# Low parts of wk on VectorE, the second k turned straight after outB, and v loads issued from GpSimd

## The chip, the cores and the metric

One core of one Trainium2 chip runs the whole program. The metric is the device time of one execution in microseconds.

## The reference, cut to what matters

All of it is float32. Eight batches of 576 tokens go through three blocks in a row.

```python
def sm_attn(qq, kk, vv):                       # per batch and head, head_dim 64, 8 heads
    s = scale * qq @ kk.T
    a = exp(s - max(s)); a = a / (sum(a) + 1e-9)
    return a @ vv
p_packed = sm_attn(p, k, v)                    # p: 32 packed queries per head
x = sm_attn(q, p_packed, p_packed)             # [8, 576, 512]
x_prev = shift x by one token
xk = mu_k * x + (1 - mu_k) * x_prev            # the same with mu_r for xr
kk = relu(xk @ w_k)                            # 512 -> 1024
x = sigmoid(xr @ w_r) * (kk * kk @ w_v)        # 1024 -> 512
u = x + (x^T U V)^T                            # U, V of rank 32 over the 576 tokens
out = u + relu(u @ w_ch1) @ w_ch2              # 512 -> 2048 -> 512
```

## The kernel before, in words

Every large matmul is made from three passes over split operands: a value is kept as a high part (rounded to the faster format, written by ScalarE) and a low part (the value minus the high part, one subtraction on VectorE or GpSimd), and hi*hi, hi*lo and lo*hi are accumulated (L883, L908, L922).

The engines run fixed lists of items, in the same order on each engine; an item does on an engine what it has to do there, and semaphores join them (`everything`, L1423).

**First items** (`first_items`, L190). Attention of batch 0 alone: k turned on TensorE (`k0`), then the steps `scores1`, `a`, `pv`, `pp`, `scores2`, `sm1`, `norm0`, `norm1`, `outA`, `outB`. `scores2` and `sm1` turn the second scores of two halves of the heads, take maxima and subtract them on VectorE (L795 to L801), ScalarE takes the exponential (L737); `norm0` and `norm1` sum, invert, scale and turn (L806 to L817) for the matmuls of `outA` and `outB` (L713), whose results are copied into x by ScalarE and VectorE (L743, L823). Between these steps the high parts of the weights of the second block are cast by ScalarE (items `w`, L1804), one chunk of 128x1024 at a time, from five staging slots: 10 chunks, 4 of wk, 2 of wr, 4 of wv. GpSimd makes the low part of each in four pieces (L1707), then loads the next chunk into the free slot (`load_w`, L1682). After `outB` come the mix of x and its shifted copy (L848, L861), its split (L873, L880), and `k1`: the rows of k of batch 1, loaded by SyncE, are turned on TensorE (L556, L563) and copied by ScalarE and VectorE (L618, L632). TensorE also runs filler transposes of the identity whose result nobody reads (`idle_turns`, L1742), as many as the table IDLE_TURNS (L80) says: 24 at the start, 112 after `scores2` and 36 after `outB` of batch 0.

**Second block with attention beside it.** Four pairs of batches, three chunks of 384 tokens each. A chunk is 17 slots (L61): 8 groups `k`, 3 groups `r`, 6 halves `v`, each of 12 matmuls. The attention steps of coming batches are laid into slots by tables (`batch_plans`, L98): in the first pair, those of batch 1 by the table `second`, of batches 2 and 3 by `third` and `fourth`. The first `k` group waits until all low parts of wk exist, the first `r` group for two chunks more, the first `v` group for all ten (L1763). After each group, ScalarE and VectorE empty the bank and square, split or multiply (L943, L932, L972, L960, L956, L983). A finished x2 tile is turned by VectorE (L991) and stored to a scratch in DRAM by SyncE, four issues a tile (L1605); x2 tiles 0 and 2 of a chunk go through one buffer, so the turn of tile 2 waits for the store of tile 0 (L990).

Loads stand in the same item lists, on SyncE's queue: k and q of a coming batch (L1467), p (L1474), and `load_v` (L1476) one batch ahead: ten issues, eight heads and four tails gathered in two, placed one slot after the `pv` step (L683) that reads the old rows, for which it waits.

GpSimd's list (L1697 to L1736): the low parts of the ten chunks, `scale_p` (L1676) for each batch, and in between the early pieces of the third block's weights: load a piece (L1385 to L1391), which waits for VectorE's low part of the piece before, and make its sums (L1397 to L1402); ScalarE then casts it at a fixed slot (`e_hi`, L1414), VectorE makes the low part (L1419), SyncE stores it.

**Third block.** Five column pairs of tokens; per pair two halves g, each with a stage of products into the hidden layer (L1178) and a stage of products out of it (L1266), by a scheme with seven products (R11 to T4) in three banks a side. Between products VectorE adds what a bank holds to acc (`dve_sum`, L1323). At the end of a pair eight tiles are turned by VectorE (`dve_turn_out`, L1343) and stored by SyncE, at the very end by SyncE and ScalarE. In the last stage of all, acc of two tiles is first added into the bank of product T4 (`dve_last`, L1305), TensorE's T4 waits for that (L1263), and the last two turns read the bank itself.

Of the kernel before, what the change touches and what calls it, by code (L numbers as in the profile page):

```python
# [78 lines left out]

IDLE_TURNS = {"first": 24, (0, "scores2"): 112, (0, "outB"): 36}  # L80

# [16 lines left out]
def batch_plans(kind):  # L98


    if kind == FIRST:
        third = batch_slots(15, 17, 20, 22, 23, 24, 25, 26, 28, 29, 31, 34, 36)
        fourth = batch_slots(37, 38, 40, 42, 43, 44, 45, 46, 47, 49, 50, 53, 55)
    else:
        third = batch_slots(6, 8, 11, 13, 15, 16, 17, 19, 21, 23, 25, 28, 30)
        fourth = batch_slots(32, 33, 35, 37, 38, 39, 40, 42, 45, 47, 50, 53, 55)
    here = (3, {at: steps for at, steps in fourth.items() if at < CHUNKS * NSLOT})
    rest = (1, {at - CHUNKS * NSLOT: steps for at, steps in fourth.items() if at >= CHUNKS * NSLOT})
    if kind == FIRST:
        second = {0: ("scores1",), 2: ("a",), 4: ("pv", "qA"), 5: ("qB",), 7: ("pp",), 8: ("scores2",),  # L110
                  9: ("sm1", "norm0"), 10: ("norm1",), 12: ("outA",), 13: ("outB",)}
        return [(1, second), (2, third), here]
    return [rest, (2, third), here] if kind == MIDDLE else [rest]
# [76 lines left out]
def first_items():  # L190

    items = [("start_loads",), ("p0",), ("k0",)]
    nw = 0
    for step in UNIT_STEPS[UNIT_STEPS.index("scores1"):]:
        if step in ("qA", "qB"):
            continue
        items.append(("attn", 0, step))
        if step == "scores1":
            items += [("load_k1",), ("load_p", 1), ("load_z", 1, 2), ("load_z", 1, 3)]
        elif step == "pv":  # L200
            items += [("load_v", 1), ("q0", 1)]
        elif step == "pp":
            items.append(("q0_tails",))
        elif step == "norm1":
            items.append(("omu",))
        elif step == "a":
            items.append(("q0", 0))
        for _ in range(WEIGHTS_AFTER.get(step, 0)):
            items.append(("w", nw))
            nw += 1  # L210
    items += [("mix", 0, 0), ("split", 0, 0), ("k1",)] + [("w", i) for i in range(nw, NWA - 2)]
    items += [("attn", 1, "p"), ("load_p", 2)]
    return items
# [49 lines left out]

def last_stage(p, g):

    return p == NB - 1 and g == NG - 1


def pair_plan(p, left, turns):
# [3 lines left out]
    for g in range(NG):  # L273
# [27 lines left out]
        for e in range(NPROD * NU):  # L301
# [10 lines left out]
            if i == NU - 1 and pos == R11:  # L312
                items += [("seed", g, 0), ("seed", g, 1)]
            elif i == NU - 1:
                if not (pos == T4 and last_stage(p, g)):
                    ready += [[("sum", p, g, SUM_AT[one])] for one in READY[pos]]
                if g == NG - 1 and pos in (R21, T3, R22):
                    pair = TILES[2 * (pos - R21):2 * (pos - R21) + 2]
                    done = [[("turn", p, TILES.index(t)), ("out", p, TILES.index(t))] for t in pair]
                    if p == NB - 1:  # L320
                        ready += done
                    else:
                        turns += done
            if last_stage(p, g) and pos == R22 and i in (1, 2):
                items.append(("last", i - 1))
            if g == NG - 1 and p < NB - 1 and e in US_AT:
# [29 lines left out]
class Attention:  # L356


    def __init__(self, sb, sem, scope):
# [26 lines left out]
        self.k1_act, self.k1_dve = sem("k1_act"), sem("k1_dve")  # L386
        self.v0_in, self.v1_in, self.v_in = sem("v0_in"), sem("v1_in"), sem("v_in")
        self.kq_ok, self.p_scaled, self.pT_ok = sem("kq_ok"), sem("p_scaled"), sem("pT_ok")
# [13 lines left out]
def build(nc, q, k, v, p, mu_k, mu_r, w_k, w_v, w_r, u, vv, w1, w2, out):  # L402
# [89 lines left out]
    w_in = [sem(f"w_in{i}") for i in range(RA)]  # L492
    w_hi, w_lo = sem("w_hi"), sem("w_lo")
    scaled_prev, mix_ok, x_hi, x_lo = sem("scaled_prev"), sem("mix_ok"), sem("x_hi"), sem("x_lo")
# [24 lines left out]
    hid_hi, hid_lo = sem("b_hid_hi"), sem("b_hid_lo")  # L519
    sum_ok, turn_ok, last_ok = sem("b_sum_ok"), sem("b_turn_ok"), sem("b_last_ok")  # L520
    out_done = [sem(f"b_out_done{i}") for i in range(2)]
# [122 lines left out]
    def pe_attn(pe, n, step):  # L644
# [29 lines left out]
        elif step == "pv":  # L674
            if n < 2:
                pe.wait_ge((L.v0_in, L.v1_in)[n], 16 * 3)
            else:
                pe.wait_ge(L.v_in, VLOADS * 16 * (n - 1))
            for hp in range(2):
# [185 lines left out]
    def act_split(act, C, which, sides=(0, 1)):  # L865
        if not (isinstance(C, int) and C == 0):
            act.wait_ge(moe_ps, MOE_GROUPS * (C - 1) + (KR if which else NFA))
        if isinstance(C, int) and C == 0 and which == 1:
            act.wait_ge(w_lo, NWA - 2)
        for side_ in sides:  # L870
# [63 lines left out]
    def act_group(act, C, c, slot):  # L934
# [11 lines left out]
        else:  # L946
# [5 lines left out]
            if isinstance(C, int) and C == 0 and at == 0:  # L952
                act.wait_ge(u_split, 1)
                act.wait_ge(w_lo, NWA)
            ge(act, x2s_lo, TPC * (C - 1) + at + 1)
# [289 lines left out]
    def pe_m2(pe, p, g, pos, i):  # L1245
# [6 lines left out]
        if i == 0:  # L1252
# [6 lines left out]
            else:  # L1259
                read = {T3: T2, R22: T1, T4: T3}[pos]  # L1260
                pe.wait_ge(sum_ok, base + SUM_AT[READY[read][-1]] + 1)
                if pos == T4 and last_stage(p, g):
                    pe.wait_ge(last_ok, 2)  # L1263
        for j in range(2):
# [32 lines left out]

    def dve_last(dve, j):

        p, st, w = NB - 1, 2 * (NG * NB - 1) + 1, PAIRS_B[NB - 1][1]  # L1300
        dve.wait_ge(sum_ok, sum_no(p, NG - 1, SUM_AT["22", "X", j]) + 1)
        dve.wait_ge(sum_ok, sum_no(p, 0, SUM_AT["21", "X", j]) + 1)
        nt, half = sum_place("21", j)
        to = role(st, j, "X")[:, 0:w]
        nc.vector.tensor_tensor(to, to, acc[p % 2][:, nt, half, 0:w], ALU.add).then_inc(last_ok, 1)  # L1305

    def sum_place(out_, j):
# [17 lines left out]
    def dve_turn_out(dve, p, k):  # L1325
        w = PAIRS_B[p][1]
        out_, j = TILES[k]
        no = len(TILES) * p + k
        if k >= 6 and p == NB - 1:
            dve.wait_ge(prod_ps, entry(p, NG - 1, T4, NU - 1, 1) + 1)  # L1330
        else:
            dve.wait_ge(sum_ok, sum_no(p, NG - 1, SUM_AT[(out_, LAST_SUM[out_], j)]) + 1)
        if no == 0:
# [5 lines left out]
        nt, half = sum_place(out_, j)  # L1339
        src = acc[p % 2][:, nt, half, 0:w]  # L1340
        if k >= 6 and p == NB - 1:
            src = role(2 * (NG * p + NG - 1) + 1, j, "X")[:, 0:w]
        nc.vector.transpose(blocks(turn_place(p, k)), blocks(src)).then_inc(turn_ok, 1)  # L1343

# [130 lines left out]

    def load_v(eng, n):  # L1476
        ge(eng, att.pv_ps, n)
        for h in range(VLOADS):
            if h < H:
                src = v[n, h, 0:1, :]  # L1480
                rows = bass.AP(src.tensor, src.offset, [[(TT - 1) * D, 4], [KB * D, 32], [1, (TT - 1) * D]])
                eng.dma_start(att.vn[:, h, 0:TT - 1, :].rearrange("p t d -> p (t d)"), rows).then_inc(att.v_in, 16)  # L1482
            else:
                quad = h - H
                src = v[n, :, :, :].rearrange("h (i m) d -> i h m d", m=KB)[:, :, 4 * (TT - 1) + quad, :]
                eng.dma_start(att.vn[32 * quad:32 * quad + 32, :, TT - 1, :], src).then_inc(att.v_in, 16)

# [21 lines left out]
    def load_attn(eng, kind, n, part):  # L1509
# [5 lines left out]
        elif kind == "load_v":  # L1515
            if n == 1:
                eng.wait_ge(att.pv_ps, 1)
                load_first_v(eng, n)
            else:
                load_v(eng, n)  # L1520
        else:
# [140 lines left out]
    def _(pool):  # L1662
# [26 lines left out]
        for i, m in enumerate((mu_k, mu_r)):  # L1689
# [6 lines left out]
                       u[TAIL:S, :].rearrange("(t p) r -> p t r", p=P)).then_inc(const_in, 16)  # L1696
        for i in range(NWA):  # L1697
            _, dst, a = w_chunks[i]
            pool.wait_ge(w_hi, i + 1)
            if i == CT:  # L1700
                scale_p(1)
            if i == CT:
# [7 lines left out]
            if i + RA < NWA:  # L1710
                pool.wait_ge(w_lo, i + 1)
                load_w(i + RA)
# [6 lines left out]
        for k in range(len(FIRST_AT)):  # L1719
            early_piece(k)  # L1720
            if k == 0:
                scale_p(3)
        scale_p(4)
        for g in range(1, PAIRS - 1):
            for k in range(len(EARLY_AT)):
                early_piece(early_no(g, k))
                if k == 2:
                    scale_p(2 * g + 3)
            if 2 * g + 4 < B:
                scale_p(2 * g + 4)  # L1730
        for n in range(EARLY, PIECES):
# [9 lines left out]
    def _(pe):  # L1741
# [9 lines left out]
        def first(item):  # L1751
            if item[0] in ("p0", "k0", "q0", "q0_tails", "k1"):
                pe_first(pe, *item)
            elif item[0] == "attn":
                pe_attn(pe, item[1], item[2])
                idle_turns(IDLE_TURNS.get(item[1:], 0))

        def do_a(item, g, c):
            C = CHUNKS * g + c
            if item[0] in ("k", "r", "v"):  # L1760
                if isinstance(C, int) and C == 0 and item[1] == 0:

                    pe.wait_ge(w_lo, {"k": CT, "r": CT + CT // 2, "v": NWA}[item[0]])  # L1763
                pe_group(pe, C, c, item)
# [97 lines left out]
    def _(dve):  # L1862
# [4 lines left out]
        def first(item):  # L1867
# [6 lines left out]
            elif item[0] == "split":  # L1874
                dve_split(dve, 0, item[1])
            elif item[0] == "omu":
                dve.wait_ge(const_in, 96)
# [37 lines left out]
        def do_b(item, p):  # L1915
# [4 lines left out]
            elif item[0] == "sum":  # L1920
                dve_sum(dve, *item[1:])
            elif item[0] == "last":
                dve_last(dve, item[1])
            elif item[0] == "turn":
# [33 lines left out]
```

## Time and profile before

| | us |
|---|---|
| three runs: median (lowest to highest) | 1359.19 (1357.71 to 1361.4) |
| the profiled execution | 1359.9 |
| its span in the trace | 1358.1 |
| TensorE busy | 1318.2 (97%) |
| VectorE busy | 955.9 (70%) |
| ScalarE busy | 703.8 (52%) |
| GpSimd busy | 209.0 (15%) |
| mean granted TensorE clock, share of full speed | 0.993 |

The second block runs from about 49 us to 606, the third to the end. A row of a timeline gives start and duration of an operation or of a merged run of equal ones, and in brackets how long its engine sat idle before it and what released it. SPq and POOLq are the issues of SyncE's and GpSimd's queues. A row that begins with a stretch (215.90:222.10) gives its length and then, within it, the busy time and instructions of PE, PEld (TensorE's weight loads), DVE (VectorE), ACT (ScalarE) and POOL (GpSimd), the granted TensorE clock as a share of 2.4 GHz, the busy share of the DMA engines and GB/s.

### The profile page before, as it was taken

How to read it: one execution, taken by the hardware profiler on the slowest of the kernel's cores; microseconds unless marked ns; L12 is line 12 of the kernel's file. 1: busy time of each engine (PE TensorE's matmuls, PEld its weight loads, DVE VectorE, ACT ScalarE, POOL GpSimd, SP SyncE). 2: the span in 40 equal slices, each digit the busy share in tenths (PEclk: the TensorE clock that was granted, in tenths of full speed). 3: DMA queues.
4: the chain of work that ended last, by engine and by line, in shares of the span. 5: the costliest groups of instructions: out<-in, count | busy, mean ns of one | idle time of the engine just before them, and what ended most of it. 6: DMA issues, size and time to landing. Idle time of an engine off the chain costs nothing.

```text
span 1358.1 us, 21513 instructions
## 1 busy us (share of the span) xinstructions
PE 1318.2 (97%) x7686; PEld 1134.8 (84%) x7686; DVE 955.9 (70%) x1553; ACT 703.8 (52%) x1235; POOL 209.0 (15%) x294
## 2 busy tenths in 40 slices
PE   8889998999999999999999999999999999999997
PEld 7868877888888888888999999888888888888886
DVE  5787977787877877674568676847587566856556
ACT  4656554555555556543545554645355544645352
POOL 6621021322022203412002002000030003000000
PEclk9999998999999999999999999999999999999999
DMA  9645574757465613965888899787867887678766
GB/s 242 141 87 88 132 156 95 155 146 158 98 140 137 161 24 92 282 181 148 264 261 258 261 269 318 238 241 205 240 184 201 249 225 213 190 207 214 218 190 127
DMA packets 433496, 252.50 MB, mean 186 GB/s; under 512 B 309776, under 2 KB 353840, under 8 KB 433392
## 3 DMA queue, kind: packets, MB, share of 16 engines
q1 hardware_dynamic: 422768, 238.20, 65.6%
q0 software_dynamic: 4016, 11.82, 2.7%
q10 hardware_dynamic: 6608, 1.11, 0.5%
q8 instruction: 62, 1.02, 0.3%
q14 instruction: 42, 0.34, 0.1%
HBM read 201.25 MB, written 49.81 MB: 185 GB/s over the span
## 4 chain that ended last, share of the span: by engine, by line
PE 72%; DVE 13%; SPq 7%; issue 3%; DMA 3%; ACT 2%; POOL 1%; DVEq 0%; ACTq 0%; POOLq 0%
PE bank L1178 25%; PE bank L1266 25%; PE bank L923 7%; PE bank L909 6%; PE bank L888 4%; SPq L1467 3%; SPq L1482 2%; DVE mixed L861 2%; DVE square L972 1%; DVE k_lo L960 1%; SPq L1605 1%; DVE kqT L767 1%; DVE xr_lo L880 1%; PE bank L1745 1%; PE bank L1005 1%
## 5 line engine op out<-in xcount | busy, mean ns | idle before, releaser
L1266 PE MATMUL bank<-hid_parts,w_ring 128*128 128x512 f32 (+1 forms) x1680 | 355.0, 370 | 5.7 <-issue 2.3
L1178 PE MATMUL bank<-u_parts,w_ring 128*128 128x512 f32 (+1 forms) x1680 | 353.9, 368 | 0.8 <-DVE hid_raw L1223 0.8
L1266 PEld LDWEIGHTS bank<-hid_parts,w_ring 128*128 128x128 f32 x1680 | 304.9, 188 | 54.3 <-issue 13.1
L1178 PEld LDWEIGHTS bank<-u_parts,w_ring 128*128 128x128 f32 x1680 | 304.9, 188 | 40.6 <-issue 1.3
L1289 ACT ACTIVATE hid_parts<-hid_raw 128x512 fp32r<-128x512 f32 (+1 forms) x280 | 164.8, 589 | 143.2 <-PE bank L1266 142.3
L1295 DVE TENSOR_TENSOR hid_parts<-hid_raw,hid_parts 128x512 fp32r<-128x512 f32 (+1 forms) x280 | 179.9, 646 | 72.2 <-ACT hid_parts L1289 68.5
L909 PE MATMUL bank<-xk_hi,wk_hi 128*128 128x384 f32 x384 | 132.5, 345 | 0.9 <-DVE x L983 0.8
L909 PE MATMUL bank<-xk_lo,wk_hi 128*128 128x384 f32 x384 | 129.5, 337 | 0.0
L909 PE MATMUL bank<-xk_hi,wk_lo 128*128 128x384 f32 x384 | 129.4, 337 | 0.0
L923 PE MATMUL bank<-wv_hi,k_hi 128*128 128x512 f32 x288 | 113.7, 395 | 0.2 <-ACT x L956 0.2
L923 PE MATMUL bank<-wv_lo,k_hi 128*128 128x512 f32 x288 | 112.2, 390 | 0.0
L923 PE MATMUL bank<-wv_hi,k_lo 128*128 128x512 f32 x288 | 112.1, 389 | 0.0
L943 ACT ACTIVATE square<-bank 128x384 f32<-128x384 f32 x96 | 47.0, 490 | 115.9 <-PE bank L909 89.2
L972 DVE TENSOR_TENSOR square<-square 128x384 f32<-128x384 f32 x96 | 55.6, 579 | 59.7 <-ACT square L943 59.5
L1102 POOL TENSOR_TENSOR u_sums<-acc 128x512 f32<-128x512 f32 (+1 forms) x10 | 12.1, 1214 | 503.0 <-DVE acc L1090 503.0
L1223 DVE TENSOR_TENSOR hid_raw<-bank,hid_z 128x512 f32<-128x512 f32 (+1 forms) x40 | 25.5, 638 | 85.1 <-PE bank L1178 82.8
L909 PEld LDWEIGHTS bank<-xk_hi,wk_hi 128*128 128x128 f32 x384 | 72.8, 190 | 12.1 <-issue 4.7
L1323 DVE TENSOR_TENSOR acc<-bank,acc 128x512 f32<-128x512 f32 (+1 forms) x118 | 73.1, 630 | 7.1 <-PE bank L1266 7.0
L861 DVE SCALAR_TENSOR_TENSOR mixed<-x,mu,mixed 128x384 f32<-128x384 f32 x96 | 57.2, 657 | 28.0 <-ACT mixed L848 27.9
L909 PEld LDWEIGHTS bank<-xk_lo,wk_hi 128*128 128x128 f32 x384 | 72.7, 189 | 1.1
L909 PEld LDWEIGHTS bank<-xk_hi,wk_lo 128*128 128x128 f32 x384 | 72.6, 189 | 0.0
L923 PEld LDWEIGHTS bank<-wv_hi,k_hi 128*128 128x128 f32 x288 | 54.0, 188 | 16.1 <-issue 4.0
(176 smaller groups left out, 1929.7 us busy)
## 6 DMA issues: line engine op xcount, KB each, us to landing
w_ring<-w_parts SPq DMA_DIRECT2D x560, 256.0 KB, 3.7
w_parts<-early_out SPq DMA_DIRECT2D x23, 896.0 KB, 5.1
x_scratch<-x SPq DMA_DIRECT2D x144, 64.0 KB, 2.1
kq_parts<-in_q SPq DMA_DIRECT2D x112, 72.0 KB, 2.4
w_parts<-piece_out SPq DMA_DIRECT2D x9, 896.0 KB, 4.6
kq_parts<-in_k SPq DMA_DIRECT2D x96, 72.0 KB, 2.8
v_rows<-in_v SPq DMA_DIRECT2D x49, 128.0 KB, 5.5
x_tiles<-x_scratch SPq DMA_DIRECT2D x6, 1024.0 KB, 7.1
```

The source lines that it names most:

```text
L861: last = nc.vector.scalar_tensor_tensor(out3, segments(c, ft, 0), mu[:, which, ft:ft + 1], out3, ALU.mult, ALU.add)
L888: last = nc.tensor.matmul(bank, a, b_, start=(done == 0), stop=(done == 3 * n_terms - 1))
L909: last = nc.tensor.matmul(bank[:, 0:CHUNK], wk[a][:, ct, at * P:(at + 1) * P], xk[b_][:, ct, :], start=(ct == 0 and a == 0 and b_ == 0), s ...
L923: last = nc.tensor.matmul(bank, k2[a][:, f, at * P:(at + 1) * P], wv[b_][:, f, :], start=(f == 0 and a == 0 and b_ == 0), stop=(f == NFA - ...
L943: nc.scalar.activation(square[:, at % 2, :], bank[:, 0:CHUNK], ACT.Relu).then_inc(k_ev, 1)
L972: nc.vector.tensor_tensor(square[:, at % 2, :], square[:, at % 2, :], square[:, at % 2, :], ALU.mult).then_inc(squared, 1)
L1178: last = nc.tensor.matmul(to, wring[:, e % RW, ct, a, :], uc[:, pos, b, ct, 0:w], start=(pos in FRESH and ct == 0 and a == 0 and b == 0), ...
L1266: last = nc.tensor.matmul(role(st, j, BANK_OF[pos])[:, 0:w], wring[:, e % RW, j, a, :], hid[:, no % RH, b, 0:w], start=(pos in FRESH and i ...
L1289: nc.scalar.activation(hid[:, no % RH, 0, 0:w], raw[:, pos, i, 0:w], ACT.Copy).then_inc(hid_hi, 1)
L1295: nc.vector.tensor_tensor(hid[:, no % RH, 1, 0:w], raw[:, pos, i, 0:w], hid[:, no % RH, 0, 0:w].bitcast(F32), ALU.subtract).then_inc(hid_l ...
L1323: nc.vector.tensor_tensor(to, role(st, j, name)[:, 0:w], to, ALU.add).then_inc(sum_ok, 1)
L1467: eng.dma_start(part[32 * quad:32 * quad + 32, :, :], src).then_inc(done, 16)
```

## The change

It has these parts. The low parts of wk move from GpSimd to VectorE: four subtractions of 128x1024 as items `wk_lo`, after `pp`, `norm1`, `outA` and `outB` of batch 0, with a semaphore of their own; GpSimd only waits for each and loads the next chunk. The fillers after `outB` go, so that `k1` follows `outB` on TensorE at once; 24 fillers stand behind `k1`, and the 112 after `scores2` become 104. In the table of batch 1 the steps from `scores2` on come one slot later. The v rows of batches 3 to 7 are issued from GpSimd's queue: batch 3 after the first early piece, batch 4 after the fourth, batches 5 and 7 after the fourth piece of their pair, batch 6 after the eighth, before `scale_p`. The addition of acc into the bank in the last stage goes: its sums are made as in every other stage, and the last two turns read acc.

```diff
-IDLE_TURNS = {"first": 24, (0, "scores2"): 112, (0, "outB"): 36}
+IDLE_TURNS = {"first": 24, (0, "scores2"): 104, "k1": 24}
...
-        second = {0: ("scores1",), 2: ("a",), 4: ("pv", "qA"), 5: ("qB",), 7: ("pp",), 8: ("scores2",),
-                  9: ("sm1", "norm0"), 10: ("norm1",), 12: ("outA",), 13: ("outB",)}
+        second = {0: ("scores1",), 2: ("a",), 4: ("pv", "qA"), 5: ("qB",), 7: ("pp",), 9: ("scores2",),
+                  10: ("sm1", "norm0"), 11: ("norm1",), 13: ("outA",), 14: ("outB",)}
...
         elif step == "pp":
-            items.append(("q0_tails",))
+            items += [("q0_tails",), ("wk_lo", 0)]
         elif step == "norm1":
-            items.append(("omu",))
+            items += [("wk_lo", 1), ("omu",)]
+        elif step in ("outA", "outB"):
+            items.append(("wk_lo", 2 + int(step == "outB")))
...
             elif i == NU - 1:
-                if not (pos == T4 and last_stage(p, g)):
-                    ready += [[("sum", p, g, SUM_AT[one])] for one in READY[pos]]
+                ready += [[("sum", p, g, SUM_AT[one])] for one in READY[pos]]
...
-            if last_stage(p, g) and pos == R22 and i in (1, 2):
-                items.append(("last", i - 1))
...
-                if pos == T4 and last_stage(p, g):
-                    pe.wait_ge(last_ok, 2)
...
-        if k >= 6 and p == NB - 1:
-            dve.wait_ge(prod_ps, entry(p, NG - 1, T4, NU - 1, 1) + 1)
-        else:
-            dve.wait_ge(sum_ok, sum_no(p, NG - 1, SUM_AT[(out_, LAST_SUM[out_], j)]) + 1)
+        dve.wait_ge(sum_ok, sum_no(p, NG - 1, SUM_AT[(out_, LAST_SUM[out_], j)]) + 1)
...
-    def load_v(eng, n):
+    def load_v(eng, n, done):
...
-            else:
-                load_v(eng, n)
+            elif n == 2:
+                load_v(eng, n, att.v2_in)
...
-        for i in range(NWA):
+        for i in range(CT):
+            pool.wait_ge(wk_lo_ok, i + 1)
+            load_w(i + RA)
+        scale_p(1)
+        for i in range(CT, NWA):
             _, dst, a = w_chunks[i]
             pool.wait_ge(w_hi, i + 1)
-            if i == CT:
-                scale_p(1)
             if i == CT:
                 pool.wait_ge(x_lo, 2)
...
             early_piece(k)
             if k == 0:
                 scale_p(3)
+                load_v(pool, 3, att.v_in)
+        load_v(pool, 4, att.v_in)
         scale_p(4)
         for g in range(1, PAIRS - 1):
             for k in range(len(EARLY_AT)):
                 early_piece(early_no(g, k))
                 if k == 2:
                     scale_p(2 * g + 3)
+                if k == 3:
+                    load_v(pool, 2 * g + 3, att.v_in)
             if 2 * g + 4 < B:
+                load_v(pool, 2 * g + 4, att.v_in)
                 scale_p(2 * g + 4)
...
             if item[0] in ("p0", "k0", "q0", "q0_tails", "k1"):
                 pe_first(pe, *item)
+                idle_turns(IDLE_TURNS.get(item[0], 0))
...
-                    pe.wait_ge(w_lo, {"k": CT, "r": CT + CT // 2, "v": NWA}[item[0]])
+                    if item[0] == "k":
+                        pe.wait_ge(wk_lo_ok, CT)
+                    else:
+                        pe.wait_ge(w_lo, {"r": CT // 2, "v": NWA - CT}[item[0]])
...
+            elif item[0] == "wk_lo":
+                i = item[1]
+                dve.wait_ge(w_hi, i + 1)
+                nc.vector.tensor_tensor(wk[1][:, i, :], stage_a[i], wk[0][:, i, :].bitcast(F32),
+                                        ALU.subtract).then_inc(wk_lo_ok, 1)
```

## Rows read from the trace of the kernel before

**Rows 1.** The page's busy times, share of the span and instructions of each engine.
```profile
PE 1318.2 (97%) x7686; PEld 1134.8 (84%) x7686; DVE 955.9 (70%) x1553; ACT 703.8 (52%) x1235; POOL 209.0 (15%) x294
```

**Rows 2.** The timeline of all engines, 23 to 49 us.
```profile
23.37 12.45 PE L1745 MATMUL bank<-ident 128*128 128x128 f32 x112
...
27.72 2.33 DVE L801 TENSOR_TENSOR probs<-probs,tok_max 128x576 f32<-128x576 f32 x1
...
30.75 2.55 DVE L809 TENSOR_SCALAR tok_sum<-tok_sum 128x18 f32<-128x18 f32 x1
...
38.56 0.75 PE L713 MATMUL bank<-kqT,packed 32*64 32x288 f32 x16 [2.74 <-DVE kqT L817]
...
40.99 5.82 PE L1745 MATMUL bank<-ident 128*128 128x128 f32 x36
...
45.42 1.95 DVE L880 TENSOR_TENSOR xk_lo<-mixed,xk_hi 128x768 fp32r<-128x768 f32 x2
...
48.87 0.45 PE L909 MATMUL bank<-xk_hi,wk_hi 128*128 128x384 f32 x1
```

**Rows 3.** Two lines' instructions on VectorE: shortest, median and longest duration in ns.
```profile
L801 DVE TENSOR_TENSOR probs<-probs,tok_max x16: 757/758/2332, 25.1 to 491.3; 128x576 f32<-128x576 f32 x16
...
L809 DVE TENSOR_SCALAR tok_sum<-tok_sum x16: 175/177/2547, 30.8 to 504.5; 128x18 f32<-128x18 f32 x16
```

**Rows 4.** The timeline of VectorE, GpSimd and TensorE, 56 to 77 us.
```profile
56.27 1.09 DVE L960 TENSOR_TENSOR k_lo<-square,k_hi 128x384 fp32r<-128x384 f32 x1
...
68.18 3.17 POOL L1707 TENSOR_TENSOR wv_lo<-stage_x,wv_hi 128x256 fp32r<-128x256 f32 x4 [2.44 <-ACT wv_hi L1804]
...
76.25 1.21 PE L700 MATMUL bank<-kqT,packedT 64*32 64x288 f32 x32 [2.58 <-ACT packedT L733]
```

**Rows 5.** Timelines of SyncE's queue, VectorE and TensorE, 192 to 216 us; then busy times, PEclk, DMA.
```profile
192.60 9.29 SPq L1482 DMA_DIRECT2D v_rows<-in_v  x8
...
203.90 10.20 SPq L1605 DMA_DIRECT2D x_scratch<-x  x12
...
211.43 0.71 DVE L991 STREAM_TRANSPOSE x<-x 128x512 f32<-128x512 f32 x1 [3.36 <-DMA x_scratch<-x]
...
215.99 0.69 PE L1005 MATMUL bank<-x2s_hi,u_tiles 128*64 128x512 f32 x1 [5.48 <-DVE x2s_lo L1016]
...
215.90:222.10 6.20, 6.11 (x30) 4.50 (x31) 3.66 (x7) 2.38 (x4) 1.44 (x2) 0.50 0.10 36
```

**Rows 6.** Timelines of GpSimd, TensorE and ScalarE, 257 to 279 us.
```profile
257.30 0.72 POOL L1386 DMA_DIRECT2D early_raw<-in_moe_w_ch  x1 [4.36 <-issue]
...
259.01 1.32 PE L683 MATMUL bank<-v_rows,probs 128*32 128x64 f32 x80
...
261.54 0.46 POOL L1402 TENSOR_TENSOR early_raw<-early_raw 128x128 f32<-128x128 f32 x1
...
264.43 0.56 POOL L1389 DMA_DIRECT2D early_raw<-in_moe_w_ch  x1 [2.43 <-DVE early_out L1419]
...
265.53 0.71 POOL L1391 DMA_DIRECT2D early_raw<-in_moe_w_ch  x1
...
270.89 0.86 POOL L1402 TENSOR_TENSOR early_raw<-early_raw 128x128 f32<-128x128 f32 x1
...
278.12 0.94 ACT L1414 ACTIVATE early_out<-early_raw 128x896 fp32r<-128x896 f32 x1
```

**Rows 7.** Timelines of TensorE and VectorE, 1319 us to the end; then busy times and PEclk.
```profile
1319.70 22.83 PE L1266 MATMUL bank<-hid_parts,w_ring 128*128 128x512 f32 x100
...
1344.42 7.29 PE L1266 MATMUL bank<-hid_parts,w_ring 128*128 128x512 f32 x24 [1.89 <-DVE bank L1305]
...
1348.11 1.28 DVE L1323 TENSOR_TENSOR acc<-bank,acc 128x512 f32<-128x512 f32 x2
...
1351.76 1.54 DVE L1343 STREAM_TRANSPOSE acc<-bank 128x512 f32<-128x512 f32 x2 [0.93 <-PE bank L1266]
...
1345.10:1348.50 3.40, 3.40 (x10) 2.61 (x9) 1.38 (x3) 0.63 (x1) 0.00 (x0) 0.50 0.71 121
```

More of the change, by code:

```diff
@@ L261 @@
 TURN_AT = (5, 11, 17, 23)
-def last_stage(p, g):
-    return p == NB - 1 and g == NG - 1
 def pair_plan(p, left, turns):
@@ L386, in __init__ @@
         self.k1_act, self.k1_dve = sem("k1_act"), sem("k1_dve")
-        self.v0_in, self.v1_in, self.v_in = sem("v0_in"), sem("v1_in"), sem("v_in")
+        self.v0_in, self.v1_in, self.v2_in, self.v_in = sem("v0_in"), sem("v1_in"), sem("v2_in"), sem("v_in")
         self.kq_ok, self.p_scaled, self.pT_ok = sem("kq_ok"), sem("p_scaled"), sem("pT_ok")
@@ L492, in build @@
     w_in = [sem(f"w_in{i}") for i in range(RA)]
-    w_hi, w_lo = sem("w_hi"), sem("w_lo")
+    w_hi, wk_lo_ok, w_lo = sem("w_hi"), sem("wk_lo_ok"), sem("w_lo")
     scaled_prev, mix_ok, x_hi, x_lo = sem("scaled_prev"), sem("mix_ok"), sem("x_hi"), sem("x_lo")
@@ L519, in build @@
     hid_hi, hid_lo = sem("b_hid_hi"), sem("b_hid_lo")
-    sum_ok, turn_ok, last_ok = sem("b_sum_ok"), sem("b_turn_ok"), sem("b_last_ok")
+    sum_ok, turn_ok = sem("b_sum_ok"), sem("b_turn_ok")
     out_done = [sem(f"b_out_done{i}") for i in range(2)]
@@ L676, in pe_attn @@
                 pe.wait_ge((L.v0_in, L.v1_in)[n], 16 * 3)
+            elif n == 2:
+                pe.wait_ge(L.v2_in, 16 * VLOADS)
             else:
-                pe.wait_ge(L.v_in, VLOADS * 16 * (n - 1))
+                pe.wait_ge(L.v_in, VLOADS * 16 * (n - 2))
             for hp in range(2):
@@ L868, in act_split @@
         if isinstance(C, int) and C == 0 and which == 1:
-            act.wait_ge(w_lo, NWA - 2)
+            act.wait_ge(w_lo, NWA - CT - 2)
         for side_ in sides:
@@ L953, in act_group @@
                 act.wait_ge(u_split, 1)
-                act.wait_ge(w_lo, NWA)
+                act.wait_ge(w_lo, NWA - CT)
             ge(act, x2s_lo, TPC * (C - 1) + at + 1)
@@ L1296, in dve_split2 @@
                                 ALU.subtract).then_inc(hid_lo, 1)
[L1298 to L1305, printed above, removed]
     def sum_place(out_, j):
@@ L1339, in dve_turn_out @@
         nt, half = sum_place(out_, j)
[L1340 to L1343, printed above, removed]
+        nc.vector.transpose(blocks(turn_place(p, k)), blocks(acc[p % 2][:, nt, half, 0:w])).then_inc(turn_ok, 1)
     def turn_place(p, k):
@@ L1481, in load_v @@
                 rows = bass.AP(src.tensor, src.offset, [[(TT - 1) * D, 4], [KB * D, 32], [1, (TT - 1) * D]])
-                eng.dma_start(att.vn[:, h, 0:TT - 1, :].rearrange("p t d -> p (t d)"), rows).then_inc(att.v_in, 16)
+                eng.dma_start(att.vn[:, h, 0:TT - 1, :].rearrange("p t d -> p (t d)"), rows).then_inc(done, 16)
             else:
@@ L1485, in load_v @@
                 src = v[n, :, :, :].rearrange("h (i m) d -> i h m d", m=KB)[:, :, 4 * (TT - 1) + quad, :]
-                eng.dma_start(att.vn[32 * quad:32 * quad + 32, :, TT - 1, :], src).then_inc(att.v_in, 16)
+                eng.dma_start(att.vn[32 * quad:32 * quad + 32, :, TT - 1, :], src).then_inc(done, 16)
     def load_first_rows(eng, src, to, h, done, n=0):
@@ L1518, in load_attn @@
                 load_first_v(eng, n)
-            else:
-                load_v(eng, n)
+            elif n == 2:
+                load_v(eng, n, att.v2_in)
         else:
@@ L1710, in _ @@
             if i + RA < NWA:
-                pool.wait_ge(w_lo, i + 1)
+                pool.wait_ge(w_lo, i - CT + 1)
                 load_w(i + RA)
@@ L1921, in do_b @@
                 dve_sum(dve, *item[1:])
-            elif item[0] == "last":
-                dve_last(dve, item[1])
             elif item[0] == "turn":
```

## The prediction

> **What bounds the kernel now.** I read the busy times first: TensorE is busy for 1318.2 of 1358.1 us, so its gaps are 40 us in all [rows 1]. A change that leaves its matmuls alone can gain only in those gaps, in filler transposes, and in stretches at the lower clock. The timeline of TensorE alone then shows where its idle spells lie; the large ones are in the prologue, at 76, at 216 and at 1344 us, and the edits meet all four.
>
> In the prologue [rows 2] the attention of batch 0 is one chain through VectorE. Two of its operations are far too long there: a subtraction of 2.33 us at 27.72 and a tiny scalar operation of 2.55 us at 30.75, where their usual times are 0.76 and 0.18 [rows 3]. GpSimd computes the low parts of wk just then. TensorE waits 2.74 us for that chain before outA, runs 36 filler transposes from 40.99 (5.82 us), turns the second k behind them and starts the first expert group at 48.87.
>
> At 76.25 it waits 2.58 us for the turned packed rows before scores2 of batch 1 [rows 4]. At 215.99 it waits 5.48 us, and the granted clock is then 0.50, the 1.2 GHz level, for 6.2 us [rows 5]. The cause stands two steps back: VectorE could not turn an x2 tile before 211.43, since the store of an earlier tile was not done (3.36 us); that store was issued at 203.90, behind ten v loads that held SyncE's queue from 192.60, 11.3 us. In the last stage TensorE waits 1.89 us at 1344.42 for VectorE's addition into its bank, then works at 0.50 of the clock for 3.4 us [rows 7].
>
> **The sum, part by part,** made against the profiled execution (1359.9 us, span 1358.1), which is 0.7 above the median of the three runs (1359.19).
>
> *Prologue.* GpSimd's four wk pieces go away: the excess of the two long operations is (2.33 - 0.76) + (2.55 - 0.18) = 3.9 us [rows 2, 3], which brings the end of the softmax chain from 38.5 to 34.6. The fillers are next: 104 instead of 112 from 23.37, at 12.45/112 = 0.111 us, end at 34.9. So outA starts at 34.95 instead of 38.56, 3.6 earlier. VectorE gains four subtractions of 128x1024. For 576 elements the trace has 0.76, for 768 half of 1.95 = 0.98 [rows 2, 3], so by that slope 1.26 each, 5.0 in all. The first lies before scores2 and costs some 0.1, covered by TensorE's fillers. The second and the small one_minus_mu run beside outA and hold the copy up by about 0.2. The third stands between the two copies of x and costs 0.25, as outB itself takes most of that time. The fourth fits before VectorE's mix, which waits for ScalarE. Queued behind them are only these copies and the mix. The split x then arrives 3.6 - 0.45 = 3.1 earlier: the first half at 46.4 - 3.1 = 43.3, all at 44.3. The second copy of x, which follows outB at 41.0 and ended near 41.9, ends at 38.8. There TensorE turns the second k at once, which takes 48.87 - 46.81 = 2.1, and runs 24 fillers, 2.7: the expert groups start at 43.7, and the second half of x is needed a microsecond later. That is 48.87 - 43.7 = 5.2. If the turning and the fillers fall at the lower clock (the 36 took 0.16 each, partly there), it is 4. I take **4.8**, as the copies of k meet the later weight casts on ScalarE. GpSimd's own queue is now loads only in this stretch, three of them later than before, at some 36, 38 and 40, for casts that stand behind the second k on ScalarE, past 44; the low parts of wr start with the split x, 3.1 earlier.
>
> *Second batch one slot later.* A sigmoid group of twelve matmuls of 128x512, 12 x 0.228 = 2.7 us at the rate of the last stage [rows 7], goes ahead of scores2. It fills the gap of 2.58; the later steps of that batch move by one slot too, so the data have the time they had. I take **2.4**; nothing at all is the low end, if VectorE, slowed by GpSimd until 71.4 (1.09 us for 384 elements, more than 768 cost elsewhere [rows 2, 4]), brings its part later still.
>
> *v loads.* Each is ten issues. SyncE loses 11.3 us of queue time per batch; the store that stood at 203.90 goes out at about 192.6, and the transpose of 211.43 no longer waits. VectorE is busy with batch 3's normalising after that, so TensorE still waits 5.48 - 3.36 = 2.1 us; 3.36 is what the wait gives. At the lower clock it lost half of 6.2, 3.1 us; a wait of 1.89 in the last stage cost one spell of 3.4 us at that level [rows 7], 1.7, so I take 1.4 of it back: **4.8**, between 3.4 (the clock falls for as long) and 8.5 (the wait is gone). The other batches' v loads lie where TensorE does not wait long; **0.3**, between one worse and three better, since TensorE's gaps there are short but ScalarE, VectorE and the queues run close together.
>
> On GpSimd's side the ten issues cost 0.56 for a head (128 rows) and 0.71 for a tail [rows 6]: 8 x 0.56 + 2 x 0.71 = 5.9 us. Behind them in the queue is the next piece of the expert weights, for which ScalarE waits, and behind ScalarE TensorE's banks. For batch 5: v is read by 260.3, GpSimd is free at 262.0; its loads end at 267.9, and the next piece takes what it took from 264.43 to 271.75, 7.3: 275.2, against ScalarE's cast at 278.12. Nothing, with 2.9 us to spare.
>
> The Trainium skill, "DMA: Bandwidth & Descriptors", section "Issuing engines are not separate DMA queues", holds that issuing from several engines saves only the sequencer's time, usually small beside the transfer. By that rule the 4.8 would be near nothing; the rows speak against it here, since what waited was a store behind 11.3 us of issuing.
>
> *Last stage.* The addition of acc into the bank goes. TensorE's last 24 matmuls start at 1342.5, not 1344.42, and at 22.83/100 = 0.228 take 5.5 instead of 7.29: the end of TensorE moves by 1.9 + 1.8 = 3.7. In their place two sums (1.28 [rows 7]) stand behind the last matmul and ahead of the last two turns, 1.52 as before. Net **2.4**. Nothing else is late next: what TensorE would wait for, the sums of the step before, stands ahead of the removed additions on VectorE.
>
> Sum: 4.8 + 2.4 + 4.8 + 0.3 + 2.4 = 14.7 us; 1359.9 - 14.7 = 1345.2 profiled, **1344.5** against the median.
>
> **Rivals.** *VectorE takes the prologue back* (0.14). Until 71 us its operations are slowed while GpSimd makes the other low parts [rows 4], and it comes only 3.1 earlier where TensorE is 4.8 earlier. Then 1.7 of the first term and most of the second are lost: 14.7 - 4.1 = 10.6, 1348.6. For it: VectorE has hardly a gap there. Against it: the last low part, at 68.18, waited 2.44 us for ScalarE's cast, so GpSimd has room.
>
> *The SyncE relief is worth little* (0.12). The chain at 208 to 216 is VectorE's own as soon as the store is gone; if something else of it is late and the clock falls as long as before, half of 4.8 stays, and the prologue gives 4: 11.5, 1347.7.
>
> *More than forecast* (0.05): the wait at 216 goes wholly, 3.7 more, 1340.8.
>
> *GpSimd becomes late, slower than before* (0.07). The place is the piece behind the v loads of batches 5 and 7. By the spare above, ten issues may take 8.8 us, 0.88 each; SyncE's took 1.16 on average for the heads (9.29/8), which would be 3 us late and mostly absorbed. The loss outweighs the gain when each batch is 7.5 late, at 1.6 us per issue. The dearest issue in the trace is the one at 257.30, 0.72 with a pause of 4.36 ahead of it, 5.1: at that price ScalarE would be 42 us late, twice, less some 4 that the banks absorb: 1344.5 + 77 = 1421. For it: such a pause exists. Against it: the issues of the next piece, seven microseconds later, cost 0.56 and 0.71.
>
> The Trainium skill, "SBUF — State Buffer", section "SBUF: two separate sides", says that a DMA issued by GpSimd can be locked out of writing descriptors while VectorE runs certain operations, and gives 3.1 us for one that alone takes 0.6. By its figure, as an estimate, the piece would come 22 us late twice, near 1380; in this trace the issue at 264.43 ran in 0.56 beside VectorE's subtraction.
>
> **The numbers.** Forecast 0.62 (own range 1341.5 to 1348), the rivals 0.14, 0.12, 0.05, 0.07. About 0.3%, 4.1 us, is what a measurement of this kernel can tell from no change. The range 1340.5 to 1350 holds the forecast and three rivals' centres with the bounds of the prologue (1 us) and the store (3.7 up, 1.4 down). Faster: all but the slow rival and a little of the two weak ones, 0.91; same 0.04; slower 0.05.
>
> **What would show it.** Right: VectorE's two long operations at 0.8 and 0.2; outA near 35 and the first expert group at 43 to 45; no idle spell ahead of scores2 of batch 1; SyncE's stores of x2 with no v load ahead of them, and TensorE's wait near 200 at about 2 us with one short spell at 1.2 GHz; the last 24 matmuls without a gap at 0.23 us each, then two sums and two turns. Wrong: ScalarE waiting for GpSimd ahead of the casts of the pieces behind the v loads of batches 5 and 7, a first group later than 46, or a wait near 200 that is as long as now.

## The result and the profile after

The kernel before took 1360.82 us in ten runs beside the changed one (1357.71 to 1363.23), the changed kernel 1353.22 (1349.93 to 1356.64): ratio 0.995, interval 0.9936 to 0.9963. It is faster, by 7.6 us between the medians (6.8 by the ratio) and not by the 14.7 forecast, and outside the range. The profiled execution took 1356.26, 3.0 over the median of its kernel, so its trace shows less of the gain than the runs do: its span is 1354.4, 3.7 less than before. TensorE's mean granted clock in it is 0.989 where it was 0.993.

The page's busy times, against [rows 1], and its line of the granted clock by fortieths of the span:

```profile
PE 1317.4 (97%) x7666; PEld 1134.1 (84%) x7666; DVE 955.6 (71%) x1557; ACT 700.7 (52%) x1233; POOL 227.9 (17%) x328
...
PEclk9999999989999999999999999999999999999999
```

GpSimd has 18.9 us more of work and TensorE's total has hardly fallen, though fillers went: some of it ran at half clock. The timeline of VectorE and then that of TensorE, 22 to 46 us, against [rows 2, 3]:

```profile
22.23 1.23 DVE L1869 TENSOR_TENSOR wk_lo<-stage_r,wk_hi 128x1024 fp32r<-128x1024 f32 x1 [1.15 <-ACT wk_hi L1794]
...
27.24 0.76 DVE L797 TENSOR_TENSOR probs<-probs,tok_max 128x576 f32<-128x576 f32 x1
...
28.70 0.18 DVE L805 TENSOR_SCALAR tok_sum<-tok_sum 128x18 f32<-128x18 f32 x1
...
35.49 0.74 PE L709 MATMUL bank<-kqT,packed 32*64 32x288 f32 x16
...
39.00 3.45 PE L550 MATMUL bank<-ident,k_rows 128*128 128x128 f32 x16 [1.01 <-ACT x L739]
...
45.36 0.42 PE L905 MATMUL bank<-xk_hi,wk_hi 128*128 128x384 f32 x1
```

The two long operations are gone and outA starts 3.1 us earlier. The first expert group starts 3.5 earlier, not 5.2: the turn of k takes 3.45 us at a clock of 0.50, where it takes 1.91 to 1.94 at full clock in runs below.

The timelines of TensorE and of SyncE's queue near 200 us, against [rows 5]:

```profile
194.41 12.90 SPq L1584 DMA_DIRECT2D x_scratch<-x  x12
...
209.19 0.56 PE L1001 MATMUL bank<-x2s_hi,u_tiles 128*64 128x512 f32 x1 [2.36 <-DVE x2s_lo L1012]
```

The stores go out 9.5 us earlier and the wait is 2.36 instead of 5.48. Then what was not there before. Timelines of GpSimd, ScalarE, TensorE and SyncE's queue, 252 to 276 us, against [rows 6], and the last two rows for batch 7:

```profile
252.63 4.86 POOL L1461 DMA_DIRECT2D v_rows<-in_v  x7 [1.15 <-PE bank L679]
...
263.68 0.68 POOL L1461 DMA_DIRECT2D v_rows<-in_v  x1 [6.19 <-issue]
264.35 1.21 POOL L1465 DMA_DIRECT2D v_rows<-in_v  x2
265.56 0.57 POOL L1368 DMA_DIRECT2D early_raw<-in_moe_w_ch  x1
...
273.11 0.45 POOL L1381 TENSOR_TENSOR early_raw<-early_raw 128x128 f32<-128x128 f32 x1
...
259.61 8.56 SPq L1446 DMA_DIRECT2D kq_parts<-in_k  x8
268.21 0.72 SPq L1536 DMA_DIRECT2D w_parts<-early_out  x1
...
274.33 0.95 ACT L1393 ACTIVATE early_out<-early_raw 128x896 fp32r<-128x896 f32 x1 [4.19 <-DMA w_parts<-early_out]
...
275.71 0.80 PE L884 MATMUL bank<-wr_hi,xr_hi 128*128 128x512 f32 x1 [3.75 <-ACT square L939]
...
412.69 0.68 POOL L1461 DMA_DIRECT2D v_rows<-in_v  x1 [5.99 <-issue]
...
424.35 0.77 PE L884 MATMUL bank<-wr_hi,xr_hi 128*128 128x512 f32 x1 [3.30 <-ACT square L939]
```

Busy times of the stretches behind the two waits, the granted clock ahead of the DMA share:

```profile
275.70:282.00 6.30, 6.29 (x17) 4.96 (x18) 6.16 (x11) 2.18 (x5) 1.79 (x3) 0.58 0.52 170
...
424.30:428.00 3.70, 3.65 (x9) 2.91 (x10) 3.63 (x7) 1.92 (x5) 1.34 (x2) 0.54 0.10 34
```

The v load holds GpSimd from 252.63 to 265.56, 12.9 us, with a pause of 6.19 ahead of its eighth issue; the pause stands in every one of the changed kernel's v loads (7.82, 7.81, 6.19, 7.71 and 5.99 us). ScalarE has come to the cast of this piece at 270.14 (274.33 - 4.19). The piece's sums end at 273.56, 3.4 later; the store of the piece before, which went out at 268.21 behind k loads that took 8.56 us, holds the cast for another 0.8. Behind the cast stands ScalarE's emptying of a bank, and TensorE waits for that; it then works at about half the clock.

Starts of steps on TensorE, in us against the kernel before, each read from the timelines of one profiled execution. The columns are scores1 of batch 1 (before at 51.18), the first group on u (101.08), scores1 of batch 4 (242.92), outA of batch 4 (291.38), outA of batch 7 (508.55), and the span. The runs are described below.

| | b1 | u | b4 | outA 4 | outA 7 | span |
|---|---|---|---|---|---|---|
| changed | -3.5 | -3.6 | -8.0 | -2.1 | +0.2 | -3.7 |
| v 5, 7 on SyncE | -4.8 | -6.1 | -12.4 | -12.7 | -11.9 | -15.0 |
| all v on SyncE | -3.6 | -5.2 | -5.6 | -5.5 | -6.9 | -9.9 |
| v behind k=4 | -3.3 | -4.6 | -10.6 | -7.2 | -6.6 | -9.6 |
| fillers at outA, outB | -5.2 | -5.4 | -11.2 | -7.0 | -5.9 | -9.0 |
| old slots | -3.8 | -0.9 | -6.9 | -1.0 | -0.4 | -3.2 |

The changed kernel had 8.0 us in hand at batch 4 and lost 5.9 at the first of the two waits. It won back 1.4, lost 5.0 at the second (from -3.4 ahead of it to +1.6 behind it, with the groups at half clock) and won back 1.4; the 3.7 at the end are the last stage and some 1.3 of the third block.

A row is one execution, and equal code does not give equal rows: the runs that differ only in what comes later reach the first group on u at -3.6, -6.1, -3.5 (the run with 5120 bytes), -5.2, -4.6 and -7.4 (the run with batch 4's v alone). What the prologue and the later slots are worth can't be read from the changed kernel's row alone.

### The profile page after: what moved, and what is told of

Read it like the earlier page. It is cut to its first block, busy times and chain, and to the rows that moved or that the text cites. A ratio compares the mean times of both kernels' runs of the same rounds, so it can differ in the third digit from the quotient of the medians.

```text
span 1354.4 us, 21458 instructions
## 1 busy us (share of the span) xinstructions
PE 1317.4 (97%) x7666; PEld 1134.1 (84%) x7666; DVE 955.6 (71%) x1557; ACT 700.7 (52%) x1233; POOL 227.9 (17%) x328
## 4 chain that ended last, share of the span: by engine, by line
PE 73%; DVE 6%; SPq 6%; DMA 2%; issue 2%; ACT 1%; POOL 0%; DVEq 0%; ACTq 0%
PE bank L1174 25%; PE bank L1260 25%; PE bank L919 8%; PE bank L905 6%; PE bank L884 6%; SPq L1446 4%; SPq L1584 1%; DMA w_parts<-early_out 1%; DVE mixed L857 1%; PE bank L1001 1%; PE bank L1073 1%; DVE kqT L763 1%; PE bank L709 1%; DVE xr_lo L876 1%; DMA x_scratch<-x 0%
```

## The experiments

All times are medians; "before" is that kernel's in the same runs, 1359.86 for the first four, 1360.49 for the next four and 1360.69 for the last three.

**v of batches 5 and 7 back on SyncE's queue.**

```diff
+V_BY_SYNC = (2, 5, 7)
-            elif n == 2:
+            elif n in V_BY_SYNC:
                 load_v(eng, n, att.v2_in)
...
+        if by_pool and n in V_BY_SYNC:
+            return
```

> The changed kernel with the v rows of batches 5 and 7 issued by SyncE again; 3, 4 and 6 stay with GpSimd. Theory A (GpSimd's v loads hold back the next piece of expert weights, ScalarE waits for it, TensorE behind ScalarE): both new waits of TensorE (3.75 us at 275.7 and 3.30 at 424.4, each followed by 1.2 GHz) are gone, the stretch from 267 to 437 us costs 10.7 us less, and the time is 1353.2 - 10 = 1343 (1341 to 1346). Rival B (the v rows' transfers crowd the DMA engines beside the k rows, whoever issues them): the waits stay at half or more, 1348 to 1353. The wait near 209 stays at about 2.4 in both.

1344.89 (1343.72 to 1345.23), ratio 0.9889 [0.987, 0.9908]: 8.3 us under the changed kernel and 15.0 under the kernel before. Both waits are gone, and the cast of the same piece runs with no wait. This is the number of the forecast, met by the kernel without a part of one of its edits. Timeline of GpSimd in this run:

```profile
255.63 0.69 POOL L1382 TENSOR_TENSOR early_raw<-early_raw 128x128 f32<-128x128 f32 x1
269.39 0.55 POOL L1369 DMA_DIRECT2D early_raw<-in_moe_w_ch  x1 [13.06 <-DVE early_out L1399]
```

GpSimd has 13.06 us with nothing to do, but one piece later than where the change puts the v load.

**Room for the descriptors of GpSimd's DMAs: 5120 and 2048 bytes instead of 4096.**

```diff
-dynamic_dma_scratch_size=4096
+dynamic_dma_scratch_size=5120   # the other: 2048
```

> The changed kernel with 5120 instead of 4096 bytes of room for GpSimd's DMA descriptors. If the pause of 6 to 8 us ahead of the eighth v issue is a full descriptor room, it moves to the ninth or tenth issue or shrinks by 1 to 3 us, GpSimd's pieces come that much earlier and the time falls by 1 to 5 us against the changed kernel. If the pause has another cause (fetching of instructions, a lock by VectorE), it stays ahead of the eighth issue with the same length, and the time is the same.

> The changed kernel with 2048 bytes of room for GpSimd's DMA descriptors. Full room: a pause ahead of about the fourth v issue and another later in each batch, each load_v at 18 us or more, TensorE's waits near 275 and 424 longer, the time 1355 to 1370. Another cause: nothing moves, 1353.

1350.86 (ratio 0.9936 [0.9914, 0.9959]) and 1367.14 (1.0061 [1.004, 1.0081]). GpSimd's timeline with 5120 bytes, then GpSimd's and TensorE's with 2048:

```profile
252.63 5.45 POOL L1461 DMA_DIRECT2D v_rows<-in_v  x8 [1.25 <-PE bank L679]
258.07 1.20 POOL L1465 DMA_DIRECT2D v_rows<-in_v  x2
...
266.21 0.72 POOL L1370 DMA_DIRECT2D early_raw<-in_moe_w_ch  x1 [5.84 <-issue]
```

```profile
252.93 2.11 POOL L1461 DMA_DIRECT2D v_rows<-in_v  x3
259.70 2.02 POOL L1461 DMA_DIRECT2D v_rows<-in_v  x3 [4.67 <-issue]
266.42 1.34 POOL L1461 DMA_DIRECT2D v_rows<-in_v  x2 [4.69 <-issue]
...
280.30 0.80 PE L884 MATMUL bank<-wr_hi,xr_hi 128*128 128x512 f32 x1 [9.76 <-ACT square L939]
```

So the pause goes with the size of the room: three heads go out ahead of it with 2048 bytes and seven with 4096; with 5120 all ten issues of this batch run in 6.7 us and the pause comes ahead of the thirteenth, the piece's third load, later than was expected. Issues in a row are not the whole of it: with 2048 bytes there is a like pause behind one load, the first in 16 us,

```profile
247.83 0.72 POOL L1365 DMA_DIRECT2D early_raw<-in_moe_w_ch  x1 [4.43 <-issue]
```

and the kernel before has 4.36 us behind one load at 257.30 [rows 6] and 4.58 behind two at 385.39. What sets those isn't shown. With the smallest room TensorE waits 9.76 and 8.82 us. But with the largest it still waits 3.04 and 1.52: there the k loads take 9.41 us of SyncE's queue, the store goes out at 269.12, and the cast waits for it until 273.63, after sums that ended at 271.1. The sums came 2.4 us earlier and the cast only 0.7: once the pause is shorter, the store holds the cast. The median is 2.4 us under the changed kernel's, which the two intervals don't tell from nothing.

**All v on SyncE's queue, the rest of the change kept** (V_BY_SYNC = (2, 3, 4, 5, 6, 7)).

> The changed kernel with every v load on SyncE as before the change; the prologue, the slots of batch 1 and the last stage stay changed. The traces of the two kernels put the prologue at -3.5, the slots near 0, the last stage at -2.5: 1360.8 - 6 = 1355 (1353 to 1357). The wait of 5.5 us near 212 with 6 us at 1.2 GHz is back, those at 276 and 424 are gone. Against e1 it is 7 to 8.5 us slower (what the store behind batch 4's v rows costs). If it is as fast as e1, the gain at 216 was not the v load of batch 4.

1349.71 (1347.15 to 1351.53), ratio 0.9925 [0.9904, 0.9945]. Near 210 us the wait of before is back:

```profile
210.22 0.69 PE L1002 MATMUL bank<-x2s_hi,u_tiles 128*64 128x512 f32 x1 [4.88 <-DVE x2s_lo L1013]
```

Against the first run the relief is worth 4.8 us, the forecast's term, and less than the 7 to 8.5 expected here. Against the changed kernel it shows what the whole v edit was worth as made: 3.5 us lost. The time is 5 us under what was expected from the changed kernel's trace. The three other parts of the change, which are all that is left here, give 10.2 us (by the interval 7.5 to 13.1), where the prediction had 4.8 + 2.4 + 2.4 = 9.6.

**v of 5 and 7 by GpSimd, one piece later.**

```diff
-                if k == 3:
+                if k == 4:
                     load_v(pool, 2 * g + 3, att.v_in)
```

> The changed kernel, but GpSimd issues v of batches 5 and 7 one piece later: behind piece k=4 of the pair instead of k=3. In the run with v of 5 and 7 back on SyncE, GpSimd stood idle for 13.06 us behind the sums of that piece (256.3 to 269.39), so the 13 to 14.5 us of a v load nearly fit there, and its pause costs nobody a cast. Theory A (what the changed kernel loses at 275 and 424 us is the order on GpSimd's queue, the piece behind the v load): both waits go, 1343.5 to 1346, as with v back on SyncE or better by the 10 us of SyncE's queue. Theory B (it is v's descriptors beside the k loads that slow the store of the piece before, wherever v stands): the k loads still take 8.5 us and a wait of 2 to 3 us stays or moves to the next piece, 1349 to 1353.

1347.29 (1345.74 to 1350.32), ratio 0.9905 [0.989, 0.9919]. In between: 5.9 of the 8.3 us come back by the order alone. The pause is still 6.60 us, the k loads take 6.22 again, but ScalarE's cast and TensorE wait for the store of the piece, which took 8.6 us to land among the v rows (ScalarE's and TensorE's timelines):

```profile
270.08 0.95 ACT L1393 ACTIVATE early_out<-early_raw 128x896 fp32r<-128x896 f32 x1 [2.27 <-DMA w_parts<-early_out]
...
271.46 0.50 PE L884 MATMUL bank<-wr_hi,xr_hi 128*128 128x512 f32 x1 [2.10 <-ACT square L939]
```

Theory A holds for the larger part. Of B the wait for the store is left, without the slow k loads. The 2.4 us to the first run are inside the two intervals; the waits of 2.10 and 1.97 us in the trace are what speaks for them.

**Fillers in the two idle spells of the prologue.**

```diff
-IDLE_TURNS = {"first": 24, (0, "scores2"): 104, "k1": 24}
+IDLE_TURNS = {"first": 24, (0, "scores2"): 104, (0, "outA"): 7, (0, "outB"): 8, "k1": 24}
```

> The changed kernel with 7 filler transposes behind outA and 8 behind outB of batch 0, which fill the two idle spells of 1.01 us ahead of outB and of the second k. Theory: the clock fell at about 38.9 us because of these gaps; with the fillers it stays at 1.00, the turn of the second k takes 1.9 instead of 3.45 us, the first expert group starts at 43.8 to 44.2 instead of 45.36, the total is 1351.0 to 1352.5. Rival: VectorE and the split x set the first group anyway; then it starts at 45 and the total is the changed kernel's 1353.2 within 1 us. If the spell of 3.4 us at half clock behind 69 us stays, that is independent of this.

1352.81 (1350.44 to 1355.87), ratio 0.9945 [0.9929, 0.9962]: no difference in the total that can be told. TensorE's timeline:

```profile
38.81 1.94 PE L550 MATMUL bank<-ident,k_rows 128*128 128x128 f32 x16
...
43.67 0.42 PE L905 MATMUL bank<-xk_hi,wk_hi 128*128 128x384 f32 x1
...
58.70 1.32 PE L679 MATMUL bank<-v_rows,probs 128*32 128x64 f32 x80 [1.91 <-DMA v_rows<-in_v]
```

The clock stays at 1.00 there and the first group starts 5.2 us earlier than before, which is what the prediction had worked out for TensorE alone. Batch 1 then waits 1.91 us for v rows that have not landed, and at the first group on u it stands at -5.4.

**The last stage's edit alone, on the kernel before** (dve_last, its item and TensorE's wait for it taken out, the last two turns from acc).

> The kernel before with the last stage's edit alone (no addition of acc into the bank by VectorE ahead of T4; two sums and two turns behind the last matmul). Theory, the last term of the sum: 2.4 us, between 2.0 and 3.0, so 1357.4 to 1358.4 against 1360.2; TensorE's last 24 matmuls without a gap. Rival: the two sums and the turns behind them cost what the wait gave, then 1359.5 or more.

1358.87 (1355.98 to 1363.12), ratio 0.9995 [0.9981, 1.0008]: in the runs the gain isn't told from nothing. The trace is sharper: from the turn into out_rows to the last two turns it was 14.66 us (1337.10 to 1351.76 [rows 7]). VectorE's timeline before, and then in this run:

```profile
1337.10 0.70 DVE L1343 STREAM_TRANSPOSE out_rows<-acc 128x512 f32<-128x512 f32 x1
```

```profile
1337.39 0.70 DVE L1333 STREAM_TRANSPOSE out_rows<-acc 128x512 f32<-128x512 f32 x1
...
1348.30 1.29 DVE L1318 TENSOR_TENSOR acc<-bank,acc 128x512 f32<-128x512 f32 x2
1349.50 1.52 DVE L1333 STREAM_TRANSPOSE acc<-acc 128x512 f32<-128x512 f32 x2
```

Here it is 12.11, 2.55 less. In the changed kernel it is 12.11 too.

**The steps of batch 1 in their old slots** (the table `second` as before).

> The changed kernel with the second batch's steps in their old slots (scores2 at 8, outA at 12). Theory: the slot shift gave next to nothing, because the clock fell behind the wait of 1.84 us at 68 and took 1.7 us of what it won; with the old slots a wait of 2 to 3.5 us ahead of scores2 of batch 1 is back. Forecast of the prediction: 2.4 us slower than the changed kernel, 1355.6. If the shift is worth nothing: 1353.2 within 0.8.

1355.64 (1354.23 to 1358.75), ratio 0.9969 [0.9959, 0.9979], 2.4 over the changed kernel. TensorE's timeline:

```profile
68.12 0.33 PE L685 MATMUL bank<-ident,packed 128*128 128x128 f32 x1 [2.21 <-DVE packed L786]
73.79 2.17 PE L696 MATMUL bank<-kqT,packedT 64*32 64x288 f32 x32 [2.58 <-ACT packedT L729]
```

The wait of 2.58 is there again to the hundredth, and only 0.9 of the prologue's 3.8 us reach the first group on u.

**The fillers of before with the rest of the change** (IDLE_TURNS of before).

> The changed kernel with the fillers of before: 112 behind scores2 of batch 0, 36 behind outB and ahead of the second k, none behind it. It separates the prologue's two edits. Theory: the low parts of wk alone bring outA 2.2 to 3.0 us earlier (the last 8 fillers end 0.9 later, so up to 0.9 of the 3.1 is lost) and the first expert group comes at 46.0 to 47.5, against 45.36 in the changed kernel and 48.87 before; what the early turn adds is the rest, 1 to 2 us, and the total is 1354 to 1355.5. Rival: with VectorE as the bound behind it, batch 1's waits absorb the difference and the total is 1353.2 within 0.8.

1356.82 (1354.95 to 1364.4), ratio 0.9976 [0.9958, 0.9994]. The first expert group starts at 45.34, not at 46 or later, as the clock holds through 36 fillers and the turn takes 1.91 us: between these two executions, to that point, the early turn brought nothing (the changed code starts the group between 42.82 and 45.63 in seven executions). At scores1 of batch 4 the two still stand at the same time (234.87 and 234.88). The total is 3.6 us worse all the same, outside both expectations, with waits of 4.97 and 4.58 us where the changed kernel had 3.75 and 3.30. Why they are longer isn't shown.

**Only batch 4's v by GpSimd** (V_BY_SYNC = (2, 3, 5, 6, 7)); **and the first run with 5120 bytes and 7 fillers behind outA.**

> Only batch 4's v on GpSimd's queue; v of 3, 5, 6 and 7 on SyncE's as before. Against the run that moved 5 and 7 back (1344.9) it takes the v of 3 and 6 from GpSimd too; against the run with all on SyncE (1349.7) it leaves batch 4's alone. Theory: the whole worth of the move is the relief of SyncE at 216 us, so 1344.9 within 1 and no wait near 275 or 424. Rival: the v of 3 and 6 also relieve SyncE by something that counts, then 1346.5 to 1348.

> The run with v of 5 and 7 back on SyncE, with 5120 instead of 4096 bytes of room for the descriptors of GpSimd's DMAs, and 7 filler transposes behind outA of batch 0. Theory: the room brings nothing there, since nobody waits behind the v loads of 3, 4 and 6; the fillers hold the clock through the turn of the second k, which that run had at full clock anyway: 1344.0 to 1345.5. Rival: the fillers make batch 1 reach its v_rows before they have landed (a wait of 1.91 us at 58.70 in the run with 15 fillers), 1345.5 to 1346.5.

1345.83 (1343.92 to 1351.37), ratio 0.99 [0.9873, 0.9927], and 1345.26 (1343.56 to 1346.07), ratio 0.9885 [0.9863, 0.9907]. Both equal the first run within what the runs tell. So batch 4's v alone is enough for the relief, and neither room nor fillers bring anything that can be told once nobody waits behind a v load. The first run's kernel and the last beat both the kernel before and the changed one.

## Why the prediction was wrong

*The step that failed* is the one priced at nothing: "5.9 us", "Nothing, with 2.9 us to spare", for ten issues on GpSimd ahead of the next piece. They take 12.9 us for batch 5 and 12.8 for batch 7 (401.71 to 414.55). The issues alone would have fitted: without the pause ten run in 6.7 us, as they do with 5120 bytes. The rival on GpSimd had the scale right: lateness begins at 0.88 us per issue, and the loss outweighs the gain at 1.6. Measured are 1.29, so by its sum the place is 12.9 - 8.8 = 4.1 us late; in the trace it is 3.4, TensorE waits 3.75, and then runs at half clock. The fourth rival's mechanism came true at a price between its two marks. With it go 8.3 us: without the v loads of batches 5 and 7 on GpSimd's queue the gain is 15.0 us, where 14.7 were forecast. That the two agree to 0.3 is partly luck: in that run's trace the prologue and the slots give 6.1 to the first group on u (7.2 forecast), and from there to batch 4 it wins 6.3 (4.8 forecast). The row that showed a pause was in [rows 6], 4.36 us ahead of the issue at 257.30, and it was set aside since later issues cost 0.56 and 0.71. That row stands behind one load and so does not show how many issues fit; no row of before had ten in a row.

*What it left out:* the store of the piece before. It asked for SyncE's queue only what the change takes off it. The v rows now move beside the k loads, whose issue took 8.56 us for eight instead of the 5.99 of before, and the store stands behind them. With v on SyncE's queue the k loads took 6.34, with v one piece later 6.22; that the v rows slow them is read from these times and was not tested by itself.

*Prologue, 4.8:* the chain of VectorE came as worked out (3.6 by the fillers, 3.1 measured, the four subtractions 1.18 to 1.23 us each against 1.26). The first group came 3.5 earlier, for the clock fell in the turn of k; held up by fillers, 5.2, and in seven executions of the same code without them 3.2 to 6.1.

*Second batch one slot later, 2.4:* right, 2.4 in the runs without it. In the changed kernel's trace the two terms don't add: VectorE brought batch 1 later relative to TensorE (a wait of 1.84 us at 68.03, at half clock afterwards, where it was 0.84), as the first rival had it. That rival gave 7.2 - 4.1 = 3.1 us for both together, and this trace has 3.6. But six executions of the same code have 3.5 to 7.4, and the runs with all v on SyncE's queue speak against the rival: with it the three other parts would give 9.6 - 4.1 = 5.5 us, and they gave 10.2 (7.5 to 13.1).

*SyncE's relief, 4.8:* right, 4.8 between all v and the v of 5 and 7 on SyncE's queue, 3.9 between all v and all but batch 4's (in other runs), and 4.4 in the changed kernel's trace (from -3.6 at scores1 of batch 3 to -8.0 at that of batch 4). The Trainium skill's "DMA: Bandwidth & Descriptors", section "Issuing engines are not separate DMA queues", says that issuing from more engines saves only the sequencer's time, usually small beside the transfer. Here that time was not small: 11.3 us of issues stood ahead of a store that TensorE was waiting for.

*Last stage, 2.4:* right, 2.55 in the trace.

*GpSimd locked out by VectorE's port,* near 1380: no. The v heads run at 0.69 us each (4.86/7), and the pause went with the size of the room.

## What to carry to other kernels

Before a queue is given a burst of issues, count how many it took in a row in the trace, and look for a row with a pause: here 0.69 us an issue became 1.29 over ten. Ask where the engine is idle, not only whether there is spare before the next due time: one piece later there were 13 us. And name, for each moved transfer, the store that has to land beside it. When a trace is to price a term, look where its execution lies among the runs: this one was 3.0 us over its median.

## What was not expected of the hardware

GpSimd's v issues (128 rows of 1 KB) run at 0.69 us and then stop: after seven with 4096 bytes, for 5.0 to 9.1 us in the runs here, after three with 2048, for 4.6 to 6.8. The granted clock fell to the 1.2 GHz level behind idle spells of 1.01 us twice in a row in the changed kernel (38.5 to 41.9 us) and did not behind the same two in the run with v of 5 and 7 on SyncE. Nor does the length of the wait at 68 us settle it: 1.84 was followed by 3.4 us at half clock, 1.63 by none, but neither were 1.83 (all v on SyncE's queue) and 2.19 (v behind k=4).
